# An attention, routing and feed-forward kernel on one core: new order of the first scores, exponentials and key turn, fewer early spare products, spare products in two late waits

## The chip, the core and the metric

The kernel runs on one core of a Trainium2 chip. The metric is the device time of one execution in microseconds; the kernel before took 380.0 us (median of 3 runs, 379.94 to 380.53).

## The reference

Three stages follow each other. The first is a gated linear attention (an mLSTM) over 4 batches, 8 heads, 768 positions, 40 values per head:

```
m_new  = maximum(f + m, i)
C = exp(f + m - m_new) * C + exp(i - m_new) * v k^T
n = exp(f + m - m_new) * n + exp(i - m_new) * k
y = sigmoid(o) * (C q) / maximum(|n q|, 1)
```

The result is laid out as 3072 tokens of 320 values. The second stage is a soft mixture of 8 experts with 4 slots each: logits = x phi, softmax over tokens to fill the slots, two matrices with a ReLU between (320 to 1024 to 320), softmax over slots to combine. The third is relu(x w_in)^2 w_out with 2048 hidden values.

## The kernel before

**Tiling.** The sequence is cut into chunks of 128 positions, 6 for a batch, so that the attention has 24 steps (b, c). In a step the recurrence inside a chunk is a masked product: `decay` (L903) makes the logarithms of the decay from two small row tensors, ScalarE raises them (`decays`, L627), GpSimd (POOL) masks them (`mask`, L568), VectorE multiplies them with the scores (`weigh`, L1333), and `attend` (L944) multiplies with v. What came in from earlier chunks goes through `carry` and the faded q (`scale_q` on POOL, L561; L937 on TensorE). `add_state` (L959) makes the chunk's own state, from keys weighed on POOL (`weigh_keys`, L552 and L553). `spread_fade` (L912) makes the logarithms of the fade.

**Gates first.** All of this rests on running logarithms of the gates, which VectorE makes with scans. Part 0 holds the first third of the sequence (2 chunks), part 1 the other two thirds. For each part VectorE makes cum and src, ScalarE copies their high parts in a rounded type (`cum_high`, `src_high`), VectorE subtracts to get the low parts (`low_parts`, L1550 and L1552), and DMAs bring both into the row tensors that `decay` reads (`direct_cum`, `direct_src`, L371 and L365). `key_logs` (L1558), `raise_keyw` (ScalarE, L732), `turn_keyw` (TensorE, L1112) and `keep_keyw` (VectorE, L1564) make the key weights of a part.

**What sets the order.** Every engine runs a list written out by hand; semaphores tie them. SyncE issues most loads, in its program order: head rows, gates, constants, qk of step 0, then the direct rows of part 0, kv and qk of the next steps, the direct rows of part 1 (which wait for the low parts of part 1), then qk, kv and o of step 2 and so on. VectorE's order at the start is L1581 to L1593, ScalarE's L734 to L750, TensorE's L1120 to L1124 and then `pe_step(0, 0)`. In that step TensorE does `decay(0, 1)`, three spare products on the constants (`stay_awake(3)`, L1118, their result is read by nobody), `attend(0, 0)`, `add_state(0, 0)`, `turn_keyw(1)`, `spread_fade(0, 1)`, `score(0, 1)` (L923) and `turn_heads(0, 0)` (L969).

**The later stages.** After the attention, TensorE does the experts (L1168 to L1202), folds the combined expert output into w_in (`slot_weights`, L1238), spreads it over the partitions (`spread_weights`, L1249), and starts the last stage with half tiles (L1298), a hidden tile (L1268) and out tiles (L1288 to L1290), 6 blocks of 512 tokens.

Of the kernel before, what the change touches and what calls it, by code (L numbers as in the profile page):

```python
# [11 lines left out]
P = 128  # L12
# [39 lines left out]
def step(b, c):  # L52

    return NC * b + c
# [29 lines left out]
def build_program(nc, qk, kv, o_gate, i_gate, f_gate, phi, w1, w2, w_in, w_out, shape_constants, head_rows, out):  # L84
    with ExitStack() as ctx:
        def sb(name, shape, dt=F32, stack=ctx):
            return stack.enter_context(nc.sbuf_tensor(name, shape, dt))

        def sem(name):
            return ctx.enter_context(nc.semaphore(name))  # L90
# [5 lines left out]
        bank = [low_banks[:, i] for i in range(4)] + [heads_banks[:, i] for i in range(2)] + [high_banks[:, i] for i in range(2)]  # L96


        consts = sb("consts", [P, 2 * P])
        ident = consts[:, 0:P]  # L100
# [114 lines left out]
        heads_in = sem("heads_in")  # L215
# [119 lines left out]
        merge_bank, heads_bank, turned_bank, side_bank = bank[4], bank[5], bank[6], bank[7]  # L335
# [37 lines left out]
        def load_gates(eng, tile, gate, part):  # L373
            own = gate[:, 0:T3] if part == 0 else gate[:, T3:S].rearrange("p (u t) -> u p t", u=2)
            eng.dma_start(tile[GATES[part]], own).then_inc(gates_in[part], 16)

        def load_qk(eng, b, c):
            n, s = step(b, c), c % 3
            at_least(eng, scores, n - 2)
            at_least(eng, q_scaled, rescales(*before(b, c, 3)))  # L380
            rows = qk[b, c].rearrange("r (i q) k h t -> (r i) q (k h t)", q=FIVE)
            eng.dma_start(qk_in[0:P:2, s], rows[:, 0:FIVE - 1]).then_inc(qk_loaded[s], 16)
            eng.dma_start(qk_in[1:P:8, s], rows[:, FIVE - 1]).then_inc(qk_loaded[s], 16)
# [20 lines left out]
        def _(sp):  # L404
# [37 lines left out]
                sp.dma_start(head_rows_in[QUAD * r:QUAD * r + H], rows).then_inc(heads_in, 16)  # L442
            load_gates(sp, f_in, f_gate, 1)
            sp.dma_start(consts[:, :], shape_constants).then_inc(consts_in, 16)
            sp.wait_ge(cleared, 1)
            load_qk(sp, 0, 0)

# [40 lines left out]
            for n in range(2, STEPS):  # L488
                b, c = n // NC, n % NC
# [119 lines left out]
        def _(act):  # L609
# [10 lines left out]
            def decays(b, c, r0=0, r1=2):  # L620

                at_least(act, heads, step(b, c) - 1)
                if (b, c) == (0, 1):
                    act.wait_ge(rows_one_hot, 1)
                for r in range(r0, r1):
                    act.wait_ge(decay_logs, 2 * step(b, c) + r + 1)
                    act.activation(att_w[:, c % 2, HP * r:HP * (r + 1)],  # L627
                                   decay_bank[r][:, :].rearrange("p (h t) -> p h t", h=HP), ACT.Exp)\
                        .then_inc(decay_exp, 1)
# [86 lines left out]
            def one_hot(part):  # L716
                act.activation(row_x[0:QUAD + H, :, 2 * part:2 * part + 2], ring, ACT.Copy).then_inc(rows_one_hot, 1)

            def cum_high(part):
                own = GATES[part]  # L720
                act.wait_ge(gate_vec[part], G_CUM)
                act.activation(cum_parts[own, 0], cum[own], ACT.Copy).then_inc(gate_act[part], 1)
# [20 lines left out]
            direct_src(act, 1, 0)  # L743
            raise_keyw(0)
            one_hot(1)
            cum_high(1)
            decays(0, 0)
            src_high(1)
            act.wait_ge(v_cleared, 2)
            copy_v(0, 0)  # L750
# [138 lines left out]
        def _(pe):  # L889
# [16 lines left out]
            def spread_fade(b, c):  # L906

                pe.wait_ge(decay_exp, 2 * step(b, c) + 2)
                if (b, c) == (0, 1):
                    pe.wait_ge(pick_placed, 1)  # L910
                rows = slice(0, QUAD + H + 2)
                pe.matmul(bank[1][:, :], cum_pick[:, :, :].rearrange("p r d -> p (r d)"), row_x[rows, :, step(b, c) % ROW_RING],  # L912
                          start=True, stop=True).then_inc(fade_logs, 1)
# [163 lines left out]
            def pe_step(b, c, half, nxt=True, cur=True, prev=True, rb=None):  # L1077
                if cur and c < NC - 1 and (b, c) != (0, 0):
                    add_state(b, c, rb)
                if nxt:  # L1080
                    decay(*after(b, c))
                if (b, c) == (0, 0):
                    stay_awake(3)
                if cur:
                    attend(b, c)
                if (b, c) == (0, 0):
                    pe.wait_ge(keyw_ready, 1)
                    pe.wait_ge(cleared, 5)
                    add_state(b, c, rb)
                    turn_keyw(1)  # L1090
                if rb is not None:
                    if cur and c > 0:
                        pe.wait_ge(carry_ready, carries(b, min(c + 1, NC - 1)))
                    route(rb, c, 1 - half)
                if cur and c < NC - 1:
                    spread_fade(b, c + 1)
                if nxt:
                    score(*after(b, c))
                if prev:
                    turn_x(*before(b, c), half if c > 0 else 1 - half)  # L1100
                if cur:
                    turn_heads(b, c)
                if prev and before(b, c)[1] % TRI == TRI - 1:
                    pe.wait_ge(decay_exp, step_exps(*before(b, c)))
                    logit(*before(b, c))

            def turn_keyw(part):
                pe.wait_ge(gate_act[part], A_KEYW)
                own = GATES[part]
                for c in range(2):  # L1110
                    to = turn_ps[:, c] if part == 0 else late_turn[:, 2 + c:NC:2]
                    mm = pe.transpose(to, keyw[own, L * c:L * (c + 1)], ident[own, own])  # L1112
                mm.then_inc(keyw_turned, 1)

            def stay_awake(count, spare=heads_bank):

                for _ in range(count):
                    pe.matmul(spare[:, 0:2 * P], ident, consts[:, :], start=True, stop=True)  # L1118

            pe.wait_ge(consts_in, 16)  # L1120
            stay_awake(3)
# [34 lines left out]
            for k in range(KC):  # L1156
# [3 lines left out]
                           start=False, stop=True, skip_group_check=True)  # L1160
# [80 lines left out]
            def spread_weights(h):  # L1241
                pe.wait_ge(sw_high, h + 1)
                pe.wait_ge(sw_low, h + 1)
                for i in range(4):
                    rows = slice(QUAD * i, QUAD * (i + 1))
                    if h == 1:
                        pe.wait_ge(sw_ready[i % 2], i // 2 + 1)
                    for part in range(2):
                        mm = pe.matmul(bank[4 + i][:, 256 * h:256 * (h + 1)], spread[rows, part].rearrange("p a b s -> p (a b s)"),  # L1249
                                       sw_cols[rows, part, 256 * h:256 * (h + 1)], start=part == 0, stop=part == 1)  # L1250
                    mm.then_inc(sw_spread, 1)
# [4 lines left out]
            slot_weights(1)  # L1256
            pe.wait_ge(spread_ready, 2)
            spread_weights(0)


            def hidden_tile(tb, f, nxt=False):
# [41 lines left out]
            half_tile(1, 1).then_inc(far_h, 1)  # L1303
            half_tile(1, 0).then_inc(h_done, 1)
            spread_weights(1)

            def pe_block(tb, first=False, last=False):
                for f in range(NF):
# [15 lines left out]
        def _(dve):  # L1324
            def weigh(b, c):

                s = c % 2
                pe_read = step(b, c) + 1
                dve.wait_ge(scores, pe_read)
                for r in range(2):  # L1330
                    dve.wait_ge(decay_masked, 2 * step(b, c) + r + 1)
                    tile = att_w[:, s, HP * r:HP * (r + 1)]
                    ins = dve.tensor_tensor(tile, score_bank[r][:, :].rearrange("p (h t) -> p h t", h=HP), tile, ALU.mult)  # L1333
                ins.then_inc(weights, 1)
# [211 lines left out]
            def low_parts(part):  # L1546
                own = GATES[part]
                dve.wait_ge(gate_vec[part], G_SRC)
                dve.wait_ge(gate_act[part], A_CUM)
                dve.tensor_tensor(cum_parts[own, 1], cum[own], cum_parts[own, 0].bitcast(F32), ALU.subtract).then_inc(gate_vec[part], 1)  # L1550
                dve.wait_ge(gate_act[part], A_SRC)
                dve.tensor_tensor(src_parts[own, 1], src[own], src_parts[own, 0].bitcast(F32), ALU.subtract).then_inc(gate_vec[part], 1)  # L1552
# [8 lines left out]
            def keep_keyw(part):  # L1561
                dve.wait_ge(keyw_turned, part + 1)
                own = slice(2, NC) if part else slice(0, 2)
                dve.tensor_copy(keyw_cols[:, own], (turn_ps, late_turn)[part][:, own]).then_inc(keyw_ready, 1)  # L1564
# [23 lines left out]
            forget_logs(1)  # L1588
            source_logs(1)
            keep_keyw(0)  # L1590
            low_parts(1)
            weigh(0, 0)
            key_logs(1)  # L1593

            for c in range(NC):
# [162 lines left out]
```

## Time and profile before

| what | us |
|---|---|
| median of 3 runs | 380.0 |
| lowest, highest | 379.94, 380.53 |
| the profiled execution's own time | 380.15 |
| its span, first to last instruction | 378.4 |
| TensorE (PE) busy in it | 364.3 (96%) |
| weight loads (PEld) | 308.4 (81%) |
| VectorE (DVE) | 236.8 (63%) |
| ScalarE (ACT) | 230.3 (61%) |
| GpSimd (POOL) | 82.0 (22%) |

Busy shares are averages over stages with different limits. DVE, ACT and POOL are far from full, but each has an order, and at the start each waits for the others in turn. A busy PE is not a PE at its peak: the ends of matmuls are modelled, and its clock has two levels.

### The profile page before, as it was taken

How to read it: one execution, taken by the hardware profiler on the slowest of the kernel's cores; microseconds unless marked ns; L12 is line 12 of the kernel's file. 1: busy time of each engine (PE TensorE's matmuls, PEld its weight loads, DVE VectorE, ACT ScalarE, POOL GpSimd, SP SyncE). 2: the span in 40 equal slices, each digit the busy share in tenths (PEclk: the TensorE clock that was granted, in tenths of full speed). 3: DMA queues.
4: the chain of work that ended last, by engine and by line, in shares of the span. 5: the costliest groups of instructions: out<-in, count | busy, mean ns of one | idle time of the engine just before them, and what ended most of it. 6: DMA issues, size and time to landing. Idle time of an engine off the chain costs nothing.

```text
span 378.4 us, 9600 instructions
## 1 busy us (share of the span) xinstructions
PE 364.3 (96%) x3488; PEld 308.4 (81%) x3488; DVE 236.8 (63%) x575; ACT 230.3 (61%) x464; POOL 82.0 (22%) x124
## 2 busy tenths in 40 slices
PE   2999999999999999999899999999999999999997
PEld 1787777777777776345699999999999999999996
DVE  8577768558847855521878665565565556556553
ACT  4466677577676854120787766666666666667662
POOL 6466657456555630000000000000000000000000
DMA  2685999999798799999400020010010001001001
GB/s 78 168 259 157 279 253 276 261 264 262 217 283 243 229 343 305 363 313 327 138 1 0 2 71 0 3 69 0 0 59 11 0 0 69 0 0 69 2 0 69
DMA packets 28488, 51.49 MB, mean 136 GB/s; under 512 B 2932, under 2 KB 20180, under 8 KB 28196
## 3 DMA queue, kind: packets, MB, share of 16 engines
q1 hardware_dynamic: 25084, 40.08, 35.9%
q10 hardware_dynamic: 3368, 10.93, 9.7%
q8 instruction: 23, 0.38, 0.4%
q14 instruction: 13, 0.11, 0.1%
HBM read 46.59 MB, written 4.33 MB: 135 GB/s over the span
## 4 chain that ended last, share of the span: by engine, by line
PE 93%; ACT 2%; DMA 1%; DVE 1%; issue 1%; SPq 0%; POOL 0%; ACTq 0%; POOLq 0%
PE heads_banks L1288 7%; PE heads_banks L1289 7%; PE heads_banks L1290 7%; PE high_banks L1288 7%; PE high_banks L1289 7%; PE high_banks L1290 7%; PE low_banks L923 7%; PE heads_banks L944 6%; PE low_banks L1268 6%; PE high_banks L959 3%; PE heads_banks L937 3%; PE low_banks L903 3%; PE low_banks L978 3%; PE low_banks L1190 2%; PE high_banks L969 2%; PE low_banks L1000 2%
## 5 line engine op out<-in xcount | busy, mean ns | idle before, releaser
L840 ACT ACTIVATE relu_h<-low_banks 128x512 f32<-128x512 f32 x94 | 56.4, 600 | 59.4 <-PE low_banks L1268 59.0
L1694 DVE CAST sq_hi<-sq_h 128x512 fp32r<-128x512 f32 x94 | 40.1, 427 | 64.2 <-ACT sq_h L845 63.5
L1696 DVE TENSOR_TENSOR sq_lo<-sq_h,sq_hi 128x512 fp32r<-128x512 f32 x94 | 65.1, 693 | 3.2
L845 ACT ACTIVATE sq_h<-relu_h 128x512 f32<-128x512 f32 x94 | 59.6, 634 | 3.0
L1288 PE MATMUL heads_banks<-wo_hi,sq_hi 128*128 128x320 f32 x192 | 59.3, 309 | 0.6 <-DVE sq_lo L1682 0.6
L1289 PE MATMUL high_banks<-wo_lo,sq_hi 128*128 128x320 f32 x192 | 59.3, 309 | 0.0
L1290 PE MATMUL high_banks<-wo_hi,sq_lo 128*128 128x320 f32 x192 | 59.3, 309 | 0.0
L1288 PE MATMUL high_banks<-wo_hi,sq_hi 128*128 128x320 f32 x192 | 59.3, 309 | 0.0
L1289 PE MATMUL heads_banks<-wo_lo,sq_hi 128*128 128x320 f32 x192 | 59.2, 309 | 0.0
L1290 PE MATMUL heads_banks<-wo_hi,sq_lo 128*128 128x320 f32 x192 | 59.1, 308 | 0.0
L1333 DVE TENSOR_TENSOR att_w<-low_banks,att_w 128x512 f32<-128x512 f32 x48 | 30.9, 685 | 27.9 <-PE low_banks L923 27.9
L1289 PEld LDWEIGHTS heads_banks<-wo_lo,sq_hi 128*128 128x128 f32 x192 | 36.0, 188 | 3.8
L568 POOL TENSOR_SCALAR_AFFINE_SELECT att_w<-att_w 128x512 f32<-128x512 f32 x48 | 32.1, 691 | 30.6 <-ACT att_w L627 30.6
L1288 PEld LDWEIGHTS heads_banks<-wo_hi,sq_hi 128*128 128x128 f32 x192 | 36.0, 188 | 1.7 <-issue 0.9
L1268 PE MATMUL low_banks<-combT,sw_parts 128*128 (+1 forms) x94 | 37.2, 396 | 0.0
L1288 PEld LDWEIGHTS high_banks<-wo_hi,sq_hi 128*128 128x128 f32 x192 | 36.0, 188 | 0.0
L1290 PEld LDWEIGHTS high_banks<-wo_hi,sq_lo 128*128 128x128 f32 x192 | 36.0, 188 | 0.0
L1289 PEld LDWEIGHTS high_banks<-wo_lo,sq_hi 128*128 128x128 f32 x192 | 36.0, 188 | 0.0
L1290 PEld LDWEIGHTS heads_banks<-wo_hi,sq_lo 128*128 128x128 f32 x192 | 36.0, 188 | 0.0
L627 ACT ACTIVATE att_w<-low_banks 128x512 f32<-128x512 f32 x48 | 26.0, 595 | 16.4 <-PE low_banks L903 16.4
L923 PE MATMUL low_banks<-qk_in 64*128 64x128 f32 x384 | 32.9, 290 | 0.0
L561 POOL TENSOR_TENSOR q_fade<-qk_in,fade_b 128x512 f32<-128x512 f32 x20 | 26.2, 1309 | 23.3 <-ACT fade_b L637 23.3
(206 smaller groups left out, 556.0 us busy)
## 6 DMA issues: line engine op xcount, KB each, us to landing
w_sb<-in_w SPq DMA_DIRECT2D x8, 1280.0 KB, 12.2
w_a<-in_w ACTq DMA_DIRECT2D x16, 512.0 KB, 5.9
kv_in<-in_kv SPq DMA_DIRECT2D x24, 320.0 KB, 5.3
qk_in<-in_qk SPq DMA_DIRECT2D x24, 256.0 KB, 4.2
o_in<-in_o_gate SPq DMA_DIRECT2D x24, 160.0 KB, 5.3
out<-out_sb SPq DMA_DIRECT2D x5, 640.0 KB, 3.2
wo_raw<-in_w_out SPq DMA_DIRECT2D x4, 640.0 KB, 13.1
w_b<-in_w ACTq DMA_DIRECT2D x8, 256.0 KB, 7.0
```

Source lines behind the costliest of these rows:

```text
L561: pool.tensor_tensor(q_fade[:, s], qk_in[:, c % 3, 0], fade_b[:, fade_slot(b, c)], ALU.mult).then_inc(q_scaled, 1)
L568: pool.affine_select(out=tile, in_=tile, compare_op=ALU.is_ge, fill=0.0, base=0, pattern=[[0, HP], [1, L]], channel_multiplier=-1).then_in ...
L840: act.activation(relu_h[:, slot], bank[slot][:, :], ACT.Relu).then_inc(relu_done, 1)
L845: act.activation(sq_h[:, slot], relu_h[:, slot], ACT.Square).then_inc(sq_done, 1)
L923: mm = pe.matmul(score_bank[r][:, L * j:L * (j + 1)], qk_in[rows, s, 1, j], qk_in[rows, s, 0, j], start=True, stop=True)
L1268: pe.matmul(bank[slot][:, :], sw_parts[:, P * f:P * (f + 1)], combT[:, bass.ds(TB * tb, TB)], start=True, stop=True).then_inc(h_done, 1)
L1288: pe.matmul(o, sq_hi[:, slot, cols], wo_hi[:, f], start=f == 0, stop=False)
L1289: pe.matmul(o, sq_hi[:, slot, cols], wo_lo[:, f], start=False, stop=False)
L1290: mm = pe.matmul(o, sq_lo[:, slot, cols], wo_hi[:, f], start=False, stop=f == NF - 1)
L1333: ins = dve.tensor_tensor(tile, score_bank[r][:, :].rearrange("p (h t) -> p h t", h=HP), tile, ALU.mult)
L1694: dve.tensor_copy(sq_hi[:, slot], sq_h[:, slot]).then_inc(hi_done, 1)
L1696: dve.tensor_tensor(sq_lo[:, slot], sq_h[:, slot], sq_hi[:, slot].bitcast(F32), ALU.subtract).then_inc(lo_done, 1)
```

## The change

- SyncE waits for the head rows before it issues qk of step 0.
- ScalarE raises the first decays, `decays(0, 0)`, ahead of `cum_high(1)` instead of behind it.
- VectorE does `weigh(0, 0)` ahead of `low_parts(1)` instead of behind it.
- TensorE does one spare product instead of three in step (0, 0), and `turn_keyw(1)` behind `spread_fade(0, 1)` instead of directly behind `add_state(0, 0)`.
- TensorE does a spare product of 128 columns behind `spread_weights(0)` and one of 256 columns behind `spread_weights(1)`.

```diff
             sp.dma_start(consts[:, :], shape_constants).then_inc(consts_in, 16)
+            sp.wait_ge(heads_in, 32)
             sp.wait_ge(cleared, 1)
             load_qk(sp, 0, 0)
...
             one_hot(1)
+            decays(0, 0)
             cum_high(1)
-            decays(0, 0)
             src_high(1)
...
                 if (b, c) == (0, 0):
-                    stay_awake(3)
+                    stay_awake(1)
                 if cur:
                     attend(b, c)
                 if (b, c) == (0, 0):
                     pe.wait_ge(keyw_ready, 1)
                     pe.wait_ge(cleared, 5)
                     add_state(b, c, rb)
-                    turn_keyw(1)
...
                 if cur and c < NC - 1:
                     spread_fade(b, c + 1)
+                if (b, c) == (0, 0):
+                    turn_keyw(1)
                 if nxt:
                     score(*after(b, c))
...
-            def stay_awake(count, spare=heads_bank):
+            def stay_awake(count, spare=heads_bank, cols=2 * P):
 
                 for _ in range(count):
-                    pe.matmul(spare[:, 0:2 * P], ident, consts[:, :], start=True, stop=True)
+                    pe.matmul(spare[:, 0:cols], ident, consts[:, 0:cols], start=True, stop=True)
...
             spread_weights(0)
+            stay_awake(1, bank[0], P)
...
             spread_weights(1)
+            stay_awake(1, bank[2])
...
             keep_keyw(0)
+            weigh(0, 0)
             low_parts(1)
-            weigh(0, 0)
             key_logs(1)
```

## Rows read from the trace of the kernel before

**Rows 1.** The page, part 4: shares of the chain that ended last, by engine.

```profile
PE 93%; ACT 2%; DMA 1%; DVE 1%; issue 1%; SPq 0%; POOL 0%; ACTq 0%; POOLq 0%
```

**Rows 2.** The chain in order of time, 0 to 40 us: start, us, what.

```profile
2.76 4.67 DMA consts<-in_shape_constants
...
19.82 0.91 PE low_banks L923 x14
...
27.23 0.60 PE heads_banks L937 x16
...
32.12 0.60 PE heads_banks L937 x16
```

**Rows 3.** Timeline, all engines, 0 to 26 us: start, us, engine line op.

```profile
10.33 0.28 PEld L903 LDWEIGHTS low_banks<-row_x,row_y 10*128 10x128 f32 x2 [0.65 <-DMA row_y<-src_parts]
10.34 0.79 PE L903 MATMUL low_banks<-row_x,row_y 10*128 10x512 f32 x2
...
11.06 2.08 PE L923 MATMUL low_banks<-qk_in 64*128 64x128 f32 x16
...
11.51 1.06 ACT L627 ACTIVATE att_w<-low_banks 128x512 f32<-128x512 f32 x2
...
11.98 0.41 DVE L1550 TENSOR_TENSOR cum_parts<-cum,cum_parts 64x256 fp32r<-64x256 f32 x1
12.15 1.32 POOL L568 TENSOR_SCALAR_AFFINE_SELECT att_w<-att_w 128x512 f32<-128x512 f32 x2 [5.12 <-ACT att_w L627]
...
12.90 0.84 DVE L1552 TENSOR_TENSOR src_parts<-src,src_parts 64x256 fp32r<-64x256 f32 x1 [0.52 <-ACT src_parts L727]
...
13.67 1.27 DVE L1333 TENSOR_TENSOR att_w<-low_banks,att_w 128x512 f32<-128x512 f32 x2
...
13.79 2.93 PE L1118 MATMUL heads_banks<-consts 128*128 128x256 f32 x6
...
14.87 0.78 DVE L1558 TENSOR_TENSOR keyw_log<-src,cum 64x256 f32<-64x256 f32 x1
...
16.65 1.98 PE L944 MATMUL heads_banks<-att_w,v_one 128*64 128x128 f32 x16
...
19.37 0.47 PE L912 MATMUL low_banks<-row_x,cum_pick 42*128 42x512 f32 x1
...
22.88 1.09 PE L944 MATMUL heads_banks<-att_w,v_one 128*64 128x128 f32 x16
...
23.91 1.38 PE L923 MATMUL low_banks<-qk_in 64*128 64x128 f32 x16
```

**Rows 4.** Timeline, POOL, 11 to 32 us.

```profile
21.79 0.33 POOL L552 TENSOR_TENSOR k_w<-kv_in,keyw_cols 128x64 f32<-128x64 f32 x1
...
25.19 1.28 POOL L561 TENSOR_TENSOR q_fade<-qk_in,fade_b 128x512 f32<-128x512 f32 x1 [0.77 <-ACT fade_b L637]
```

**Rows 5.** SyncE's queue, 13 to 17 us, and the landing of the kv issued at 16.54.

```profile
13.82 1.41 SPq L365 DMA_DIRECT2D row_y<-src_parts  x2
...
16.54 0.57 SPq L416 DMA_DIRECT2D kv_in<-in_kv  x1
...
kv_in<-in_kv SPq DMA_DIRECT2D x1, 320.0 KB, 4.5
```

**Rows 6.** DMA issues at 3.8 to 4.2 us (the first qk): KB each, us to landing.

```profile
qk_in<-in_qk SPq DMA_DIRECT2D x1, 256.0 KB, 3.3
qk_in<-in_qk SPq DMA_DIRECT2D x1, 64.0 KB, 4.4
```

**Rows 7.** Timeline, PE, 177 to 188 us.

```profile
178.00 0.70 PE L1118 MATMUL low_banks<-consts 128*128 128x256 f32 x2
...
182.73 0.50 PE L1298 MATMUL low_banks<-combT,sw_parts 128*128 128x256 f32 x2 [0.46 <-ACT sw_parts L830]
183.91 0.51 PE L1268 MATMUL low_banks<-combT,sw_parts 128*128 128x512 f32 x1
185.04 0.38 PE L1288 MATMUL heads_banks<-wo_hi,sq_hi 128*128 128x320 f32 x1 [0.63 <-DVE sq_lo L1682]
```

## The prediction

> **What bounds the kernel now.** I read the shares of the chain first: TensorE (PE) holds 93% of it [rows 1]. So only what moves PE's own order of work can move the end. The chain in order of time comes next. Up to 7.43 us it goes through the landing of the constants (2.76 + 4.67), after that through PE almost alone, and the steps soon have a fixed length: the same product (L937) begins at 27.23 and at 32.12, 4.89 apart [rows 2]. Four of the five edits act before 21 us, the fifth at 182 to 185 us. What the start gains is kept only if every later step is still paced by PE, so the rows of POOL and of the SyncE queue have to be read too.
>
> The timeline of the start shows two paces on PE. The 16 instructions of a score take 2.08 us at 11.06 and 1.38 at 23.91; those of an attention product 1.98 at 16.65 and 1.09 at 22.88 [rows 3]. These are TensorE's lower level (1.2 GHz) and its upper one (2.4 GHz). The profile's clock column says 1.00 throughout, so I go by durations: the attention product ending at 18.63 is still slow, the fade product at 19.37 (0.47 us for 512 columns) is fast. The clock rose between them.
>
> **Part 1, first scores weighed ahead of later low parts, exponentials ahead of a later copy.** Today ScalarE (ACT) raises the first decays at 11.51, behind the copy of the later cum. PE's decays are there at 10.34 + 0.79 = 11.13, the first half earlier, so ACT can start near 10.8 and POOL's two masks (1.32) end near 12.75 instead of 13.47. VectorE (DVE) then waits for the scores, 11.06 + 2.08 = 13.14, and weighs from 13.2 to 14.45 (1.27 for both halves) instead of 13.67 to 14.94. Gain at the weights: 0.5 us [rows 3]. ACT's copy of cum moves from 11.19 to about 11.85; its other copies stay where they were.
>
> The price is on DVE. The two low parts (first at 11.98, 0.41 us; second at 12.90, 0.84) and the key logs (14.87, 0.78) now stand behind the weighing. The first ran mostly ahead of POOL's masks, the other two beside POOL work [rows 3]. From 14.45 POOL still weighs keys and masks [rows 4], so I let the low parts cost 0.41 to 0.84 each: the second ends at 15.3 to 16.1 instead of 13.74. That is 1.5 to 2.4 us later, and the key logs end at about 16.0 to 16.9.
>
> **Part 2, one spare product instead of three, later key turn behind the fade.** Six instructions took 2.93 us, so one product is 0.98 and two removed ones 1.95. The product now runs 13.79 to 14.77 beside the wait for the weights (14.45), and the attention product can start at 14.77 instead of 16.65: 1.88 us earlier [rows 3]. Without the cover the wait alone would give back only 0.3 more. The state product is free (kw_ready at about 13.8). The later key turn waits for the key logs and then 0.42 of ACT: 16.4 to 17.35. PE reaches it, behind attention (to 16.75), state (0.7) and fade (0.4), at 17.8. So the moved turn waits for nothing, and where it stood before it might have waited a few tenths.
>
> Of the 1.88, part is work that ran fast and would now run slow, if the clock rises at the same time. Scores of step 1 would start at 18.1 instead of 19.55. With the rise at 18.6 to 19.3 they end at 19.5 to 19.7, against 20.73 [rows 2]. I take 1.1 us gained when PE enters step 1.
>
> **Part 3, what the later low parts delay.** SyncE (SP) issues in order: two source-row DMAs (13.82, 1.41 us), then qk, kv and o of the next steps. Behind a low part that is 1.5 to 2.4 later, kv of step 2 is issued not at 16.54 but at 18.0 to 18.9. It took 4.5 us to land [rows 5], so it lands at 22.5 to 23.4 instead of 21.04. The rows themselves still suffice: issued from 15.6 to 17.6, at the 2.6 us which the first source rows took (issued about 7.7, PE released at 10.33 [rows 3]), they are there by about 19.5, against a need near 20.8. qk of step 2 (3.0 from issue to landing) comes by 21.3 against 22.8.
>
> The kv of step 2 is the tight one. POOL needs it first: keys (two instructions from 21.79, 0.9 together) and faded q (1.28) [rows 4], and between them the mask (1.32 at 12.15) [rows 3]. Begun at 22.5 to 23.4 these end 0.9 + 1.32 + 1.28 = 3.5 later, at 26.0 to 26.9. PE's L937 of step 2 starts at 27.23 now [rows 2], and with 1.1 us gained would want it at 26.1. Hence it starts at 26.1 to 27.0: **0.2 to 1.1 us** gained, and I take 0.5, toward the late end because the second low part, in a comparable place, had the 0.84. ACT has its copy of v behind the same kv (23.42 now, 23.4 then), so it keeps its old times and would alone stop the gain near 0.7. From there on loads are issued about 2 us later but needed at POOL's next keys (26.43 now) and PE paces again at 4.89 per step, so what was gained stays.
>
> **Part 4, SP waits for the head rows before the first qk.** The head rows are used at 4.78, so qk is issued at about 4.8 and 5.4 instead of 3.24 and 3.89. Its two parts took 3.3 and 4.4 from issue to landing [rows 6], giving 8.1 and 9.8, against the need at 11.06: covered with 1.2 us. Next on SP is the first cum row at 6.37, still free (4.8 + 0.6 + 0.6 = 6.0). The constants no longer share the engines with it: landing at 7.43 may become 5.5 to 7.4. That starts the first spare products earlier but not decay(0,0), which waits for the source rows until 10.33 [rows 3]; bounds for that wait are -0.3 (head rows and so the first copies a little sooner) to +0.5 (qk's packets now beside the row DMAs). I take 0. If the constants are early, PE idles about a microsecond ahead of 10.33.
>
> **Part 5, spare products in two tail waits.** A 256-column product took 0.70 us with its latency at 178.00 [rows 7]. The half-size one goes into the 0.46 us that PE waits for ACT at 182.73, about 0.3 of pace; the full one in front of the hidden tile at 183.91, whose 0.51 us then ends by about 185.0, against PE's next start at 185.04 [rows 7]. PE already ran fast behind both gaps, so nothing is to be won. I take 0, bounds -0.1 and +0.2.
>
> **Sum.** -0.5 + 0 + 0 = -0.5 us on the profiled execution's 380.15 (378.4 of span and 1.75 around it), 379.65; the same off the median of 380.0 gives **379.5**.
>
> **Rivals.** *(a) The kv is not late, or the clock rises early.* With low parts of 0.41 each, or a kv landing in 3.4 instead of 4.5, PE keeps the 1.1. If the earlier constants bring the clock up before 11 us, the first scores end 0.9 sooner, the weights 0.7 sooner (masks become the bound), and with them the low parts and the whole SP queue: 1.1 to 1.9 us, 378.1 to 378.9. For it: 1 us of extra products ahead of 10.4. Against it: products and scores from 7.48 to 16.65 did not raise it before.
>
> *(b) The clock rises later: slower.* The stretch 13.8 to 18.6, dense now with spare products, loses two of them, and PE may idle ahead of 10.33. If the next rise comes only behind the attention product of step 1, then score (2.08 against 1.38), head turns, state, decay and attention (1.98 against 1.09) run slow: 0.7 + 0.9 from these rows and as much again, estimated, for the others, about 3 us, against 1.1 gained: +1.9; if it comes at its start, +0.5. Prices 380.5 to 381.9. It decides from the point where the clock is still low at about 20.5 us, when PE would begin step 1. Against it: PE is still occupied almost without a gap from 10.33 on.
>
> The Trainium skill, "TensorE: Matmul & The Clock Gate", Part 1 (the HAM clock gate), says that activity releases the throttle and that its observation runs freely, so the point of the rise shifts from run to run. By that rule two spare products fewer can delay the rise and earlier constants advance it; rows here show only one rise, late, and three timings within 0.6 us.
>
> *(c) The gain is eaten.* kv lands at 24 or the first rows come 0.5 late: 380.0 ± 0.3. It differs from the forecast only by a few tenths.
>
> **How the numbers follow.** Forecast (0.2 to 1.1 gained) 45%, (a) 25%, (b) 15%, (c) 15%. Its own range is 378.9 to 379.8; with (a) and the near half of (b) 378.2 to 380.9. Within 0.2% (0.76 us, about what a measurement can tell from no change) lie four fifths of the forecast, (c), and a third of (b): 52%. Faster is (a) and a fifth of the forecast: 36%. Slower: 12%.
>
> **What would show it.** Part 1: the weighing (L1333) starts at 13.2, the low parts behind it at 14.5. Part 2: one product at 13.79, L944 at 14.8, the key turn at about 17.8 with no wait. Part 3: kv of step 2 issued at 18 to 19, POOL's keys of step 2 released by that DMA near 23, and PE idle in front of L937 near 26 to 27. Part 4: constants earlier than 7.4, L903 still at 10.3. Clock: the first fast row of PE; if it is a score at 11 I was too low, if L923 of step 1 takes 2 us in full I was too high. Part 5: L1288 0.4 us of pace behind an unchanged wait. A step length other than 4.89, or a wait on a DMA in a later step, would make the whole forecast wrong.

## The result and the profile after

The changed kernel took 382.25 us (median of 22 runs, 379.73 to 385.79) against 380.17 for the kernel before (22 runs, 377.98 to 382.94): **ratio 1.0058, interval 1.0036 to 1.0080**. It is slower by 2.1 us by the medians and 2.2 by the ratio; 379.5 was forecast, and the range ended at 380.9. Ratios, here and below, leave out a kernel's few slow executions (over 1.5% above its fastest); medians, ranges and counts have them all. The profiled execution took 382.05, with a span of 380.3.

The chain that ended last, by engine, is as it was, with PE one point higher:

```profile
PE 94%; ACT 2%; DMA 1%; DVE 1%; issue 1%; SPq 0%; POOL 0%; ACTq 0%; POOLq 0%
```

Timeline of the changed kernel, 0 to 32 us (start, us, engine line op). L924 is the score, L945 the attention product, L1120 the spare product, L1554 and L1556 the low parts; their line numbers before were L923, L944, L1118, L1550 and L1552. L913 is the fade product and L1337 the weighing (L912 and L1333 before):

```profile
10.95 2.08 PE L924 MATMUL low_banks<-qk_in 64*128 64x128 f32 x16
...
13.08 1.29 DVE L1337 TENSOR_TENSOR att_w<-low_banks,att_w 128x512 f32<-128x512 f32 x2 [1.25 <-PE low_banks L924]
...
13.68 1.22 PE L1120 MATMUL heads_banks<-consts 128*128 128x256 f32 x2
...
14.28 0.47 DVE L1554 TENSOR_TENSOR cum_parts<-cum,cum_parts 64x256 fp32r<-64x256 f32 x1
...
14.68 0.83 DVE L1556 TENSOR_TENSOR src_parts<-src,src_parts 64x256 fp32r<-64x256 f32 x1
...
14.84 1.98 PE L945 MATMUL heads_banks<-att_w,v_one 128*64 128x128 f32 x16
...
15.57 1.41 SPq L365 DMA_DIRECT2D row_y<-src_parts  x2
...
17.56 0.79 PE L913 MATMUL low_banks<-row_x,cum_pick 42*128 42x512 f32 x1
...
18.30 0.57 SPq L416 DMA_DIRECT2D kv_in<-in_kv  x1
18.36 2.02 PE L924 MATMUL low_banks<-qk_in 64*128 64x128 f32 x15
...
23.19 0.40 POOL L553 TENSOR_TENSOR k_w<-kv_in,keyw_cols 128x64 f32<-128x64 f32 x1 [2.86 <-DMA kv_in<-in_kv]
...
24.15 1.97 PE L945 MATMUL heads_banks<-att_w,v_one 128*64 128x128 f32 x16
...
26.05 0.55 PE L913 MATMUL low_banks<-row_x,cum_pick 42*128 42x512 f32 x1
```

The edits did what they say: weighing at 13.08, one product, first attention product at 14.84 instead of 16.65 [rows 3], and a key turn without a wait. Two things follow. PE stays at 1.2 GHz far longer: scores of step 1 take 2.02 us, the attention product of step 1 takes 1.97 where it took 1.09 [rows 3], and the fade product falls from 0.79 at 17.56 to 0.55 only at 26.05. And SyncE issues kv of step 2 at 18.30, 1.8 later than before [rows 5], so POOL waits 2.86 us for it. In this execution PE was so slow that this wait cost nothing: the chain goes through PE alone from 11 to 43 us. The chain in order of time shows what was left (L938 was L937 before):

```profile
29.44 0.60 PE heads_banks L938 x16
...
34.32 0.60 PE heads_banks L938 x16
```

This is the product that began at 27.23 and 32.12 [rows 2]: 2.2 us late, with the same step of 4.88. In the tail (timeline, PE):

```profile
184.14 0.49 PE L1120 MATMUL low_banks<-consts 128*128 128x128 f32 x2
...
184.63 0.75 PE L1301 MATMUL low_banks<-combT,sw_parts 128*128 128x256 f32 x4
...
186.94 0.39 PE L1291 MATMUL heads_banks<-wo_hi,sq_hi 128*128 128x320 f32 x1 [0.21 <-DVE sq_lo L1686]
```

The out tile (L1291) starts 1.90 later than 185.04 [rows 7], 2.31 behind the half tile (L1301) as before (185.04 - 182.73), and the span is 1.9 longer: nothing more is won or lost from there on.

### The profile page after: what moved, and what is told of

The parts are those of the page before. It is cut to its first block, busy times and chain, and to the rows that moved or that the text cites. A ratio compares the mean times of both kernels' runs of the same rounds, so it can differ in the third digit from the quotient of the medians.

```text
span 380.3 us, 9601 instructions
## 1 busy us (share of the span) xinstructions
PE 367.3 (97%) x3488; PEld 310.5 (82%) x3488; DVE 238.3 (63%) x575; ACT 229.7 (60%) x464; POOL 81.8 (22%) x124
## 4 chain that ended last, share of the span: by engine, by line
PE 94%; ACT 2%; DMA 1%; DVE 1%; issue 1%; SPq 0%; POOL 0%; ACTq 0%; POOLq 0%
PE heads_banks L1291 7%; PE heads_banks L1292 7%; PE high_banks L1293 7%; PE high_banks L1291 7%; PE high_banks L1292 7%; PE heads_banks L1293 7%; PE low_banks L924 7%; PE heads_banks L945 6%; PE low_banks L1271 6%; PE high_banks L960 3%; PE heads_banks L938 3%; PE low_banks L904 3%; PE low_banks L979 3%; PE high_banks L970 2%; PE low_banks L1192 2%; PE low_banks L1001 2%
## 5 line engine op out<-in xcount | busy, mean ns | idle before, releaser
L1291 PE MATMUL heads_banks<-wo_hi,sq_hi 128*128 128x320 f32 x192 | 59.5, 310 | 0.2 <-DVE sq_lo L1686 0.2
L1291 PE MATMUL high_banks<-wo_hi,sq_hi 128*128 128x320 f32 x192 | 59.3, 309 | 0.0
L1337 DVE TENSOR_TENSOR att_w<-low_banks,att_w 128x512 f32<-128x512 f32 x48 | 30.9, 686 | 31.4 <-PE low_banks L924 31.4
L628 ACT ACTIVATE att_w<-low_banks 128x512 f32<-128x512 f32 x48 | 26.0, 595 | 19.7 <-PE low_banks L904 19.7
L1291 PEld LDWEIGHTS heads_banks<-wo_hi,sq_hi 128*128 128x128 f32 x192 | 36.0, 187 | 1.4 <-issue 0.6
L1291 PEld LDWEIGHTS high_banks<-wo_hi,sq_hi 128*128 128x128 f32 x192 | 36.0, 188 | 0.0
L924 PE MATMUL low_banks<-qk_in 64*128 64x128 f32 x384 | 33.8, 296 | 0.0
```

What stands on the lines that cost most here:

```text
L924: mm = pe.matmul(score_bank[r][:, L * j:L * (j + 1)], qk_in[rows, s, 1, j], qk_in[rows, s, 0, j], start=True, stop=True)
L1291: pe.matmul(o, sq_hi[:, slot, cols], wo_hi[:, f], start=f == 0, stop=False)
```

## The experiments

Each ratio is to the kernel before, run beside it (185 runs of it in all, in six groups with medians 380.06 to 380.88). Each kernel ran twelve times. Its executions lie 2.7 to 9.6 us apart, so a ratio has an interval of ±0.2 to ±0.4%, and the twelve times of a kernel say more than one profile. "Three products" and "one product" are the spare products in step (0, 0); "gate order" is the place of the first weighing and the first decays.

| run | what it is | median | ratio, 95% |
|---|---|---|---|
| e1_three | changed, three products | 381.13 | 1.0032 (0.9995 to 1.0070) |
| e2_one_only | before, one product | 379.85 | 0.9973 (0.9945 to 1.0001) |
| e3_wait_tail | before, SyncE's wait and tail | 379.99 | 0.9988 (0.9963 to 1.0013) |
| e4_warm | changed, early warming | 382.37 | 1.0042 (1.0012 to 1.0072) |
| e5_no_reorder | changed, old gate order | 380.42 | 0.9984 (0.9959 to 1.0010) |
| e6_reorder_only | before, new gate order | 382.32 | 1.0033 (1.0007 to 1.0058) |
| e7_early_loads | changed, early loads | 380.39 | 0.9999 (0.9976 to 1.0021) |
| e8_one_early | before, one product, early loads | 378.57 | **0.9936** (0.9910 to 0.9962) |
| e9_early_three | e7, three products | 380.33 | 1.0002 (0.9983 to 1.0020) |
| e10_early_plain | e7, old gate order | 382.11 | 1.0010 (0.9971 to 1.0048) |
| e11_act_only | before, ScalarE's reordering | 380.30 | 0.9988 (0.9966 to 1.0011) |
| e12_dve_only | before, VectorE's reordering | 381.72 | 1.0035 (0.9992 to 1.0077) |
| e13_key_turn | e8, key turn behind the fade | 380.38 | 0.9964 (0.9923 to 1.0005) |
| e14_sp_wait | e8, SyncE's wait | 379.16 | 0.9966 (0.9928 to 1.0005) |
| e15_tail | e8, tail products | 378.69 | 0.9944 (0.9916 to 0.9972) |
| e16_act_early | e8, ScalarE's reordering | 379.15 | 0.9939 (0.9911 to 0.9966) |
| e17_key_back | e10, key turn ahead of the fade | 379.15 | 0.9966 (0.9941 to 0.9990) |
| e18_plain_three | e10, three products | 378.39 | 0.9960 (0.9941 to 0.9979) |

### Is it the clock or the loads? (e1 to e4)

The profile after names the clock, so that was the first theory. e1 puts the products back, in step (0, 0) of the changed kernel, e2 takes them out of the kernel before:

```diff
                 if (b, c) == (0, 0):
-                    stay_awake(1)
+                    stay_awake(3)
```

> The changed kernel with three spare products in step (0,0) again, all else as changed. Clock theory (two products fewer leave the clock low until 26 us): the clock rises before 20 us as in the kernel before, L945 of step 1 takes 1.1 us and not 1.97, L938 of step 2 starts near 27.2 or earlier, and the time is that of before or up to 0.5 us less, 1.6 to 2.6 us below the changed kernel. Load theory (late low parts push SyncE's queue and with it the kv of step 2): that kv still lands past 22.5 us, L938 of step 2 stays at 28 or later and the time stays 1 us or more above before.

Measured 381.13, ratio 1.0032. The clock theory asked for the time of before or less, the load theory for 1 us more; the interval holds both, and the changed kernel's as well, so e1 decides little. In its profiled execution, at 378.82 the fastest of its twelve, the clock rose early (scores in 1.16 us at 10.71) and kv of step 2 stood on the chain. Its waits (us in total, times, longest):

```profile
POOL k_w L553 <- DMA kv_in<-in_kv: 4.7, 2, 4.4
```

> The kernel before with one spare product instead of three in step (0,0), nothing else changed. Clock theory: the same late rise as in the changed kernel (first fast rows at 22 to 26 us), 1.0 to 2.5 us slower than before. Load theory: the low parts are where they were, kv of step 2 is not late, and the attention product starts up to 1.6 us earlier: 0.3 to 1.5 us faster than before.

Measured 379.85, ratio 0.9973. It is not slower, so two products fewer alone do not make the loss. A gain as the load theory has it fits (0.5 us by the medians, 1.0 by the ratio), but the interval just reaches no change. Its profiled execution was its slowest (382.36), and it shows what a late kv does once PE is early. PE's timeline, and the chain:

```profile
14.83 1.09 PE L944 MATMUL heads_banks<-att_w,v_one 128*64 128x128 f32 x16 [1.26 <-DVE att_w L1333]
...
28.41 1.97 PE L944 MATMUL heads_banks<-att_w,v_one 128*64 128x128 f32 x16
```

```profile
16.37 7.16 DMA kv_in<-in_kv
```

The clock was up before 14.83. kv of step 2, issued at 16.37, landed 7.16 us later (4.5 in the profile before [rows 5]). PE had nothing to do from 22.85 to 24.56, and behind this stop of 1.71 us the same product took 1.97: the clock had fallen. Here the clock row of the page shows it (40 slices of 9.5 us, tenths of full speed; in the third and fourth it is down):

```profile
PEclk9978999999999999999999999999999999999999
```

Asked by the microsecond, the granted clock is 0.50 from 25 to 31 us. A stop can cost its length and then a stretch at half pace. It need not: e4 below stops for 1.92 us, and its clock stays up.

e3 adds to the kernel before only SyncE's wait and the two tail products:

```diff
+            sp.wait_ge(heads_in, 32)
             sp.wait_ge(cleared, 1)
...
             spread_weights(0)
+            stay_awake(1, bank[0], P)
...
             spread_weights(1)
+            stay_awake(1, bank[2])
```

> The kernel before with only SyncE's wait for the head rows and the two spare products in the tail waits. Clock theory: three products remain, so the rise stays near 19 us; the two edits are worth 0 to -0.3 us at the start and 0 at the end: time of before within 0.4 us. Rival (these two edits cost: qk beside the first rows, and spare products that outlast their waits): 0.5 us or more slower.

Measured 379.99, 0.9988: these two edits are harmless, as expected.

e4 lets VectorE fill a tile and warms PE on it, without the constants:

```diff
+            pe.wait_ge(warm_made, 1)
+            for _ in range(6):
+                pe.matmul(heads_bank[:, 0:2 * P], headsT[:, 0, 0], headsT[:, 0].rearrange("p a t -> p (a t)"), start=True, stop=True)
             pe.wait_ge(consts_in, 16)
             stay_awake(3)
...
+            dve.memset(headsT[:, :, :, :], 0.5).then_inc(warm_made, 1)
             dve.memset(m_run[GATES[0], 0:1], -1.0e30)
```

> The changed kernel plus six spare products on a tile that VectorE fills first (so from about 1.5 us, without waiting for the constants), still one product in step (0,0). Clock theory: the clock rises before the first scores or by 15 us; the first scores take 1.0 to 1.4 us instead of 2.08, and the time is 2 to 4 us below the changed kernel and 0.5 to 2 below before. Load theory: kv of step 2 lands past 22 us as before, and the time stays within 1 us of the changed kernel.

Measured 382.37, 1.0042. In the profiled execution the clock did rise early, as the clock theory wanted, and nothing came of it. PE's timeline, and waits of POOL and PE:

```profile
14.48 1.09 PE L946 MATMUL heads_banks<-att_w,v_one 128*64 128x128 f32 x16 [1.50 <-DVE att_w L1341]
```

```profile
POOL k_w L554 <- DMA kv_in<-in_kv: 5.6, 3, 3.6
PE low_banks L905 <- DMA row_x<-cum_scratch: 1.9, 1, 1.9
PE low_banks L905 <- DMA row_y<-src_parts: 1.4, 1, 1.4
PE low_banks L925 <- DMA qk_in<-in_qk: 1.1, 1, 1.1
```

In this execution a fast PE only meets SyncE's late transfers sooner. It does not stand for its kernel, though: its mean granted clock is 1.000, and the other eleven executions have 0.982 to 0.996, so in them the clock fell again somewhere; no trace shows where. The theory was changed: VectorE's reordering holds up SyncE's queue, and the late loads stop PE.

### Which part makes the loads late? (e5, e6, e11, e12)

The order of the gate work, as in the kernel before (-) and in the changed one (+):

```diff
             keep_keyw(0)
+            weigh(0, 0)
             low_parts(1)
-            weigh(0, 0)
             key_logs(1)
...
+            decays(0, 0)
             cum_high(1)
-            decays(0, 0)
```

e5 takes both out of the changed kernel, e6 puts both into the kernel before, e11 and e12 put one each into it (decays, weighing).

> The changed kernel without its two reorderings of the gate work (VectorE weighs behind the later low parts, ScalarE raises the first decays behind the later copy, as before); one spare product, key turn behind the fade, SyncE's wait and the tail products stay. Load theory, sharpened (only the reordering makes it slower, because the later low parts hold up SyncE's queue, and kv of step 2 then stops PE): 1.5 to 3 us faster than the changed kernel, ratio to before 0.995 to 1.001. Clock theory (two spare products fewer): still 1.003 or more.

> The kernel before with only the two reorderings of the gate work; three spare products, key turn where it was. Load theory: slower than before, ratio 1.002 to 1.006; kv of step 2 is issued 1.2 us or more later than 16.54. Clock theory: three products remain, so the ratio is 1.000 or below.

> The kernel before with only ScalarE's reordering (first decays ahead of the later copy of cum). Load theory: VectorE's low parts wait a little for that copy (0.3 to 0.6 us), SyncE a little later: ratio 0.999 to 1.001. If it is ScalarE's part that costs: 1.002 or more.

> The kernel before with only VectorE's reordering (first weighing ahead of the later low parts). Load theory: this is the whole cost of the reordering, source rows issued at 15.5 or later instead of 13.82, ratio 1.002 to 1.006. If ScalarE's part costs: 0.999 to 1.001.

Measured 0.9984, 1.0033, 0.9988 and 1.0035. The first two show that the order of the gate work costs time: with the old order the changed kernel loses its loss, with the new one and all three products the kernel before gets slower. ScalarE's part is free. VectorE's is as large as both together, though its own interval still includes 1. SyncE's queue in e12 (before: 13.82 and 16.54 [rows 5]):

```profile
15.61 1.41 SPq L365 DMA_DIRECT2D row_y<-src_parts  x2
...
18.33 0.57 SPq L416 DMA_DIRECT2D kv_in<-in_kv  x1
```

### The loads moved out of the way (e7, e8, e9)

The buffers of step 2 are free from the start. So SyncE can issue these loads before it waits for the later low parts:

```diff
             load_o(0, 0)
+            load_qk(sp, 0, 2)
+            load_kv(0, 2)
             sp.wait_ge(rows_one_hot, 2)
...
                 direct_src(sp, r, 1)
-            load_qk(sp, 0, 2)
-            load_kv(0, 2)
```

> The changed kernel with one move: SyncE issues qk and kv of step 2 ahead of its waits for the later low parts (the buffers are free from the start), near 10.8 us. Load theory: kv of step 2 lands by 17 us, nobody waits for it, and 1 to 3 us of the loss go: ratio to before 0.994 to 1.001. Clock theory: no difference to the changed kernel, 1.003 to 1.008.

> The kernel before with one spare product in place of three and the same early issue of qk and kv of step 2. Load theory: in executions where the clock is high early, PE no longer stops for kv near 23 us, so 0.5 to 2 us faster than before, ratio 0.994 to 0.999. Clock theory: slower than before.

Measured 0.9999 and 0.9936. With the changed kernel the move gives back as much as was lost, and with the kernel before and one product it makes **the best version found, 2.2 us faster than before and 3.7 faster than the changed kernel** by the medians (378.57; 376.92 to 380.54). In e8 nobody but POOL, for 0.3 us, waits for a kv. The move is a gain of its own and not only a cure: e18 below has it with the old gate order and three products, and takes 0.9960. The kernel before with this move and nothing else was not run.

> The changed kernel with the early issue of qk and kv of step 2 and three spare products. It asks what the rest of the loss is once the loads are out of the way. If two products fewer delay the clock in the reordered start: below the early-loads kernel with one product, ratio to before 0.995 to 0.999, and no late rise in the profile. If the rest is the later rows and stores on SyncE's queue: no better than it, 0.999 to 1.003.

e9 is e7 with `stay_awake(3)` again. Measured 1.0002, as e7. Of the two answers offered it is nearer the second: the rest is not the products. e9 differs from e18 below in the order of the gate work alone, 1.0002 against 0.9960, so with three products some 1.6 us of the reordering's price stay with early loads. (With one product the same comparison, e7 against e10, shows none: 0.9999 against 1.0010.) The profiled execution (381.70) shows where time can go: PE's wait for rows that come back from the scratch store, further down the same queue, and the attention product behind it at half pace again. That these rows carry the 1.6 us is not shown: e13 below has the old gate order and the same stop, 2.7 us long.

```profile
PE low_banks L904 <- DMA row_x<-cum_scratch: 3.1, 1, 3.1
```

```profile
43.24 1.97 PE L945 MATMUL heads_banks<-att_w,v_one 128*64 128x128 f32 x16
```

A profile shows one execution, but the mean granted clock is on record for every execution of e1 to e18 and for 163 of the kernel before, and it tells where the clock fell again. The profiled executions with 0.991 (e2, e9, e13) each have 6 to 7 us at a granted clock of 0.50 behind a stop of PE; those with 0.999 or 1.000 have no such stretch. A late first rise does not lower the number (changed and e10: 1.000). Executions with 0.996 or less:

| loads of step 2, gate order | kernels | with a fall |
|---|---|---|
| late, old | before | 66 of 163 |
| late, old | e2, e3, e5, e11 | 6 of 48 |
| late, new | changed, e1, e6, e12 | 30 of 58 |
| early, new | e7, e9 | 5 of 24 |
| early, old | e8, e10, e13 to e18 | 10 of 96 |

The 66 of the kernel before have a median of 382.11, the other 97 one of 380.01: an execution with a fall takes some 2 us more, and in the kernel before two of five have one. The counts fit the load theory, with most falls where the loads are late in the new order and few where they are early (e13 to e16 have 6 of 48, where the kernel before, run beside them, had 19 of 35). They do not prove it: e2, e3, e5 and e11 have few as well.

### The late clock (e10, e13 to e18)

e10 is the changed kernel with both diffs above: the old order of the gate work, and the early loads.

> The changed kernel without the reordering of the gate work, with the early issue of qk and kv of step 2; one spare product, key turn behind the fade, SyncE's wait and tail products stay. Load theory: as the kernel before with one product and early loads (0.9936) or up to 0.3 us better, ratio 0.991 to 0.996, the best of all. Rival (SyncE's wait or the key turn cost something in an early clock): 0.997 or more.

Measured 1.0010 with two groups: 377.49, 377.51, 377.90, 379.03, 379.35 and seven from 382.02 to 382.95. Six of these seven have a mean granted clock of 1.000, so no fall made them slow. The load theory was wrong here: no load is late (POOL waits 0.3 us for a kv). The profiled execution, of the upper group, has the clock of the changed kernel:

```profile
24.13 1.97 PE L945 MATMUL heads_banks<-att_w,v_one 128*64 128x128 f32 x16
```

So there is a second cause after all: the late first rise, which was the first theory. The next runs add one edit at a time to e8. e13 is the key turn:

```diff
                     add_state(b, c, rb)
-                    turn_keyw(1)
...
                     spread_fade(b, c + 1)
+                if (b, c) == (0, 0):
+                    turn_keyw(1)
```

> The kernel before with one product and early loads (measured 0.9936), plus the later key turn behind the fade. If the place of the key turn brings the late clock: a good part of the executions near 382, ratio 0.998 or more. If not: 0.991 to 0.996, none above 381.

> The same kernel (before, one product, early loads) plus SyncE's wait for the head rows, which shifted PE's start by about 0.3 us (7.4 instead of 7.65, attention at 14.8 instead of 15.2). If this shift brings the late clock: a good part of the executions near 382, ratio 0.998 or more. If not: 0.991 to 0.996.

> The same kernel plus the two spare products in the tail waits. In the traces the stretch from the turn of the expert outputs to the first out tile is 8.6 us without and 8.7 with them, so 0.0 to 0.1 us: ratio 0.991 to 0.996. A ratio of 0.998 or more would make the tail a cause.

> The same kernel plus ScalarE's reordering alone (first decays ahead of the later copy). It ends the masks 0.7 us sooner, but the weighing stands behind the later low part, which then waits for ScalarE's copy: 0 to 0.4 us faster than the 0.9936, ratio 0.991 to 0.995; if the clock is what varies, 0.998.

Measured 0.9964, 0.9966, 0.9944, 0.9939. Above 382.0 lie 4 of 12 (key turn), 1 (SyncE's wait), 0 (tail) and 0 (ScalarE). Tail and ScalarE's reordering are free, and neither makes e8 faster. SyncE's wait lies between the two answers offered for it (0.9928 to 1.0005) and stays open in this kernel. The key turn is a suspect but not shown to be a cause: its profiled execution, at 382.20, had an early clock and a stop of 2.7 us for rows from the scratch, not a late clock. The last two start from e10 and put one thing back each, the key turn (e17) or the two products (e18):

> The kernel e10 (no reordering, early loads, one product, SyncE's wait, tail products) with the later key turn back ahead of the fade, where the kernel before has it. If the key turn's place helps to make the late clock: at most 2 of 12 executions at 382 or above, ratio 0.993 to 0.997. If it has no part: again about half at 382, ratio 0.999 to 1.002.

> The kernel e10 with three spare products in step (0,0) instead of one, key turn behind the fade. If the missing products help to make the late clock: no execution near 382 with a low clock at 24 us, but the two products' time is paid, ratio 0.996 to 1.000. If products have no part: again about half near 382 or above, ratio 1.001 or more.

Measured 0.9966 (377.09 to 380.80) and 0.9960 (377.12 to 381.12). Neither has one execution at 382, where e10 has seven of twelve. Both expectations of the clock held: by these runs it takes one product *and* the key turn behind the fade to make the upper group. Even then it does not come each time: e5 has both edits, and only 2 of its 12 executions lie above 382. One rival is left: e10 ran on another chip than e17 and e18 and was not run again beside them. The profiles speak against it. Of the twenty profiled executions three have a rise near 26 us (changed, e7, e10), and e7 ran on the chip of e17 and e18. They are three of the six with both edits (e4, e5 and e13 rose early); of the fourteen others none is that late. In e18, though the products cost their time, the attention product of step 1 is fast:

```profile
23.46 1.09 PE L945 MATMUL heads_banks<-att_w,v_one 128*64 128x128 f32 x16
```

## Why the prediction was wrong

- **Part 1** was right on PE's side, though it is what held up the queue (Part 3): weighing forecast at 13.2, seen at 13.08; low parts ending at 15.3 to 16.1, seen at 15.51. ScalarE's reordering alone: 0.9988.
- **Part 2** was right up to 14.84 (forecast 14.77) and for a key turn without a wait (at 18.15, forecast 17.8: state and fade were priced at 0.7 and 0.4 and took 0.81 and 0.72 on the chain, at the lower clock). The step that failed is the next, "with the rise at 18.6 to 19.3 they end at 19.5 to 19.7": I took the moment of the rise from one profiled execution and held it fixed. The scores of step 1 ended at 20.38. Rival (b) described the profile in full: a clock still low behind the attention product of step 1, "+1.9"; it was +1.9 at the out tiles. I gave it 15%, against the evidence that I had myself (two products out of the dense stretch). But (b) names only one of two conditions: the products alone (e2, e8) did no harm, nor did the key turn with three products (e18). That (b)'s price fits the one profile to a tenth is partly luck, since others of the 22 executions lie from 379.73 to 385.79.
- **Part 3** had the right transfer: kv of step 2 forecast at 18.0 to 18.9, issued at 18.30; landing forecast at 22.5 to 23.4, seen at 23.10. It failed in its effect. I let the late kv only cap a gain, because I reckoned with PE of one execution and a landing of 4.5 us. In executions with an early clock PE is 2 us and more ahead, the landing can take 7.16, PE stops, and the clock can fall behind the stop. Alone (e6) the reordering costs 0.33%, 1.3 us (0.07 to 0.58%), where at worst 0.9 less gain was forecast. And the last step, from "loads are issued about 2 us later but needed at POOL's next keys" to "what was gained stays", looked at kv alone: transfers further down the queue stop PE too (in e4 1.9 us for scratch rows and 1.1 for a qk).
- **Part 4**: with qk issued a microsecond later (4.28, forecast 4.8) the constants landed at 7.33 instead of 7.43, not at 5.5, so qk had held them up by 0.1 at most. The head rows came 0.5 earlier and with them everything up to the first scores 0.1. Forecast as 0, and about 0 (e3).
- **Part 5**: 0 forecast; 0.0 in the profile from the half tile on, and 0.9944 against 0.9936 within the noise (e15).
- **Range.** The three times that I had lay within 0.6 us and I built on them; 185 runs of the same kernel spread from 377.97 to 387.12. That spread, which I had not measured, is itself the sign that the start varies.
- **Chances.** They do not add up as written: four fifths of 45%, the 15% of (c) and a third of 15% make 56% (not 52%), (a) and a fifth of 45% make 34% (not 36%), and 10% are left for slower (not 12%).

What stays open: how often each cause acts in the changed kernel. 13 of its 22 executions have a mean granted clock of 0.996 or less, so the clock fell in them; the nine others have a median of 382.05, so falls are not all of its loss, but only one of them is profiled. With the same two edits the upper group has 2 of 12 in e5 and 7 in e10. Open too is which transfers carry the 1.6 us between e9 and e18. That late clocks fill e10's upper group is shown for its one profiled execution; for five more it is inferred from a time near 382 without a fall, and one (0.982) had a fall.

## What to carry to other kernels

Moving work ahead on one engine is paid by whoever waits for the work it overtakes: here a reordering that gives PE half a microsecond holds up a queue that issues in order, and only the transfers behind it show the price. First issue what nothing holds back (two lines moved, from 1.0058 to 0.9999; with one product in the kernel before, 0.9936), then reorder. A clock's rise read from one execution is one sample; an edit that makes the stretch before it thinner needs several executions, and their spread, before it counts as gain.

## What the runs showed of the hardware

The rise of TensorE's clock differs between executions of nearly the same start: before the first scores at 10.5 to 11.1 us (e1, e2, e4, e5, e9, e13), between 17 and 20 (before, e3, e8, e12 and most others), or near 26 (changed, e7, e10). It can fall again behind a stop: behind 1.7 us in e2, 2.7 in e13 and 3.1 in e9, each time for 6 to 7 us; behind 1.9 us in e4 it did not. The Trainium skill, "TensorE: Matmul & The Clock Gate", Part 1 (the HAM clock gate), says that the observation runs freely and that the point of the rise varies with it, by 500 ns either way from run to run. The runs here agree that it varies, but by far more: some 15 us from first to last.

The profile's granted clock shows these falls (0.50 in e2 from 25 to 31 us) but not the slow start: in the changed kernel it says 1.00 from 20 to 25 us, where the attention product takes 1.97 us, as long as in e2 at 0.50. Ahead of the first rise the durations have to be read.

The same kv transfer of 320 KB took 4.1 (e4), 4.5 (before), 4.8 (changed) and 7.16 us (e2) from issue to landing.
